# Attention with the bucket mask inside the score product, normalised probabilities and two-tile steps, in front of two feed-forward stages

## The reference

```python
B, H, S, D = q.shape                       # 2, 8, 768, 64
q_bits = (np.einsum('bhsd,dk->bhsk', q, proj) > 0)
k_bits = (np.einsum('bhsd,dk->bhsk', k, proj) > 0)
q_bucket = np.sum(q_bits * powers, axis=-1)
k_bucket = np.sum(k_bits * powers, axis=-1)
mask = q_bucket[:, :, :, None] == k_bucket[:, :, None, :]
scores = np.where(mask, q @ k.T / sqrt(D), -1e9)
scores = scores - np.max(scores, axis=-1, keepdims=True)
attn = np.exp(scores)
attn = attn / (np.sum(attn, axis=-1, keepdims=True) + 1e-09)
x = (attn @ v), heads side by side         # 1536 x 512
h = np.maximum(np.maximum(x @ w1, x @ w2), x @ w3)      # 1536 x 768
y = h @ w_out                                           # 1536 x 512
g = y @ w_in;  g = g * sigmoid(1.702 * g)               # 1536 x 2048
out = g @ w_out2
```

## Time and profile before

| | |
|---|---|
| median of 3 runs | 754.82 us (754.74 to 755.68) |
| span of the profiled execution | 752.0 us, 2.8 below the median of the runs |
| TensorE matmul (PE) busy | 740.9 us, 99% |
| TensorE weight load (PEld) busy | 638.3 us, 85% |
| VectorE (DVE) busy | 362.1 us, 48% |
| ScalarE (ACT) busy | 281.3 us, 37% |
| GpSimd (POOL) busy | 245.6 us, 33% |
| DMA, mean rate | 69 GB/s |
| mean granted clock of TensorE | 0.995 |
| attention stage | from 0 to some 280 us |

### The profile page before, as it was taken

How to read it: one execution, slowest core, us unless ns; L and a number is a source line. 1 busy time by engine, 2 the same in 40 slices (tenths; PEclk the granted TensorE clock), 3 DMA queues, 4 the chain that set the end, 5 groups by cost and what they waited for, 6 DMA issues and landing times.

```text
span 752.0 us, 12394 instructions
## 1 busy us (share of the span) xinstructions
PE 740.9 (99%) x4348; PEld 638.3 (85%) x4348; DVE 362.1 (48%) x794; ACT 281.3 (37%) x586; POOL 245.6 (33%) x230
## 2 busy tenths in 40 slices
PE   6999999999999999999999999999999999999998
PEld 5766777777677669999999999999899899989997
DVE  4988888888888872223222233232222333232222
ACT  3667676666667651111111111322222222222222
POOL 2211111211111152351455242644445445444541
PEclk8999999999999999999999999999999999999999
DMA  4422222243221141201231211212222214222112
GB/s 116 105 64 65 63 64 63 73 96 81 63 63 42 44 138 41 85 22 42 79 111 42 63 41 48 75 59 71 64 56 69 70 43 154 71 70 56 56 42 84
DMA packets 80218, 51.75 MB, mean 69 GB/s; under 512 B 28480, under 2 KB 71488, under 8 KB 80192
## 3 DMA queue, kind: packets, MB, share of 16 engines
q1 hardware_dynamic: 80192, 51.40, 25.1%
HBM read 38.80 MB, written 3.15 MB: 56 GB/s over the span
## 4 chain that ended last, share of the span: by engine, by line
PE 97%; DVE 1%; ACT 1%; DMA 1%; SPq 0%; issue 0%; DVEq 0%
PE psO L811 10%; PE psT L799 10%; PE psS L789 9%; PE psS L881 7%; PE psS L882 7%; PE psS L883 7%; PE psN L883 3%; PE psN L881 3%; PE psN L882 3%; PE psB L882 3%; PE psB L881 3%; PE psB L883 3%; PE psB L754 3%; PE psS L959 2%; PE psS L958 2%; PE psS L957 2%
## 5 line engine op out<-in xcount | busy, mean ns | idle before, releaser
L335 POOL TENSOR_SCALAR w_hi<-w_raw 128x512 fp32r<-128x512 f32 (+2 forms) x84 | 64.3, 766 | 276.1 <-PE psX L959 129.3
L358 POOL TENSOR_TENSOR w_lo<-w_raw,w_hi 128x512 fp32r<-128x512 f32 (+2 forms) x84 | 140.8, 1677 | 7.0
L417 ACT ACTIVATE probs<-masked,neg_max 128x768 f32<-128x768 f32 x96 | 89.8, 936 | 64.2 <-DVE neg_max L566 63.6
L335 POOL TENSOR_SCALAR h_hi<-h_lo 64x768 fp32r<-64x768 f32 x48 | 40.1, 835 | 209.4 <-ACT h_lo L405 204.4
L799 PEld LDWEIGHTS psT<-ident,probs 128*128 128x128 f32 x576 | 62.1, 140 | 47.6 <-issue 44.3
L566 DVE CUSTOM_DVE_ANT_0 masked<-psS,mask 128x768 f32<-128x768 f32 x96 | 91.7, 955 | 18.1 <-PE psS L789 17.7
L881 PE MATMUL psS<-x_hi,w_hi 128*128 128x384 f32 x288 | 96.6, 335 | 0.0
L883 PE MATMUL psS<-x_hi,w_lo 128*128 128x384 f32 x288 | 96.2, 334 | 0.0
L882 PE MATMUL psS<-x_lo,w_hi 128*128 128x384 f32 x288 | 96.2, 334 | 0.0
L789 PE MATMUL psS<-h_hi 128*128 128x384 f32 x384 | 93.0, 364 | 1.6 <-DVE neg_max L566 1.5
L799 PE MATMUL psT<-ident,probs 128*128 128x128 f32 x576 | 83.1, 280 | 1.5 <-ACT probs_t L425 1.5
(11 more groups left out here) (137 smaller groups left out, 1362.2 us busy)
## 6 DMA issues: line engine op xcount, KB each, us to landing
h_hi<-h_lo SPq DMA_DIRECT2D x48, 192.0 KB, 3.9
w_raw<-in_moe_w SPq DMA_DIRECT2D x36, 256.0 KB, 3.5
w_raw<-in_moe_w_in SPq DMA_DIRECT2D x32, 256.0 KB, 2.8
w_raw<-in_moe_w_out SPq DMA_DIRECT2D x32, 256.0 KB, 2.7
v_raw<-in_v SPq DMA_DIRECT2D x16, 192.0 KB, 2.4
w_raw<-in_moe_w_out SPq DMA_DIRECT2D x24, 128.0 KB, 2.4
out<-probs_t SPq DMA_DIRECT2D x12, 256.0 KB, 2.2
w_raw<-in_q SPq DMA_DIRECT2D x15, 192.0 KB, 3.3
```

The lines of the kernel that those rows point to most:

```text
L335: return pool.tensor_scalar(dst, src, 1.0, 1.0, ALU.mult, ALU.mult)
L358: pool.tensor_tensor(w_lo[par][:, c0:c1], w_raw[par][:, c0:c1], f32(w_hi[par][:, c0:c1]), ALU.subtract).then_inc(done, 1)
L417: act.activation(probs[t % 2][:, :], masked[t % 2][:, :, :].rearrange("p a b -> p (a b)"), ACT.Exp, bias=neg_max[t % 2][:, 0:1], scale=-1. ...
```

## The change

The attention stage is written anew; the loops of the feed-forward stages stay as they are.

- **Mask in the product.** The scores' second pass gets, beside the low parts, a one-hot vector of 64 buckets for queries and for keys, the latter scaled by 2^100. `project` is now one bank per head pair: four matmuls (q and k of two heads, two halves of the tokens) as four column tiles of 32. `make_bits` turns it into plus and minus one half, `spread_hot` multiplies by a table of the 64 codes, `make_hot` compares with a threshold. The separate mask, the masked scores in SBUF and the bucket numbers go.
- **Scores and exponential.** `row_max` takes the minimum straight from PSUM, and the exponential reads PSUM. There are two score pairs, `psS[0]` and `psS[1]`; each is free only when its exponential is done.
- **Normalised first.** Per two tiles VectorE makes the inverse sums (`invert_sums`), POOL scales the probabilities in place (`norm`), and only then TensorE turns them. `turn_out`, `normalise` and `turn_x` go: P*V now writes x itself, already turned, for two heads at once (the two heads are the column tiles, three query tiles of each at a time, a "unit").
- **A ring of three PSUM banks** (`psR`) takes everything that is turned or projected, in one order for the whole stage, `ring_order`.
- **Steps of two tiles**, 48 in all, six to a head pair.
- **Stacks.** Each head has four stacked operands (q and k, each with low parts and with one-hot), filled by eight DMAs of 64x768; q and k are split by POOL. SP's queue per head pair: loads of q and k of the next pair, twelve copies of high and low parts, four of one-hot, loads of v.
- POOL splits the first block of feed-forward weights in six pieces in the last pair (`early_split`).

```diff
+    ring_order = [("codes",)]
...
+    for k_ in range(STEPS + 1):
+        p_, st = k_ // 6, k_ % 6
+        if st in (3, 4) and p_ + 1 < PAIRS:
+            ring_order += [("one_hot", 2 * p_ + 2 + st - 3, j) for j in range(2)]
+        if st == 2 and p_ + 1 < PAIRS:
+            ring_order += [("bits", p_ + 1)]
+        if k_ > 0:
+            ring_order += [("probs", i, j) for i in (2 * k_ - 2, 2 * k_ - 1) for j in range(2)]
+        if st < 2 and p_ + 1 < PAIRS:
+            ring_order += [("turn", 2 * p_ + 2 + st, j) for j in range(2)]
...
@@ block.sync @@
-            def stack_qk(m, par):
-                sync.wait_ge(qk_hi_made, 2 * m + 2)
-                sync.dma_start(f32(k_st[par][0:D, :]), f32(qk_hi[D:P, :])).then_inc(qk_stacked[par], 16)
-                sync.wait_ge(qk_lo_made, 2 * m + 2)
-                sync.dma_start(f32(q_st[par][D:P, :]), f32(qk_lo[0:D, :])).then_inc(qk_stacked[par], 16)
-                sync.dma_start(f32(k_swap[par][0:D, :]), f32(qk_lo[D:P, :])).then_inc(k_swapped[par], 16)
+            def load_v(p):
+                if p >= 2:
+                    sync.wait_ge(unit_out, 2 * p - 2)
+                for a in range(2):
+                    sync.dma_start(v_raw[p % 2][a][:, :, :], v_r[2 * p + a, :, :, :]).then_inc(v_loaded[p % 2], 16)
+            def place_hi(m):
+                a = m % 2
+                if m >= 4:
+                    sync.wait_ge(scores_ready, 2 * NT * (m // 2 - 1))
+                sync.wait_ge(qk_hi_made, m + 1)
+                for rows, to, of in ((slice(0, D), Q_LO, slice(0, D)), (slice(D, P), Q_HOT, slice(0, D)),
+                                     (slice(D, P), K_LO, slice(D, P)), (slice(D, P), K_HOT, slice(D, P))):
+                    sync.dma_start(f32(stack(m, to)[rows, :]), f32(qk_hi[a][of, :])).then_inc(hi_placed[a], 16)
...
+            for p in range(PAIRS):
+                if p + 1 < PAIRS:
+                    for m in (2 * p + 2, 2 * p + 3):
+                        load_qk(m)
+                for m in (2 * p, 2 * p + 1):
+                    place_hi(m)
+                    place_lo(m)
+                for m in (2 * p, 2 * p + 1):
+                    place_hot(m)
+                if p + 1 < PAIRS:
+                    load_v(p + 1)
...
@@ block.gpsimd @@
+            for step in range(STEPS):
+                p, st = step // 6, step % 6
+                if st in (1, 2) and p + 1 < PAIRS:
+                    make_qk_hi(2 * p + 1 + st)
+                    make_qk_lo(2 * p + 1 + st)
+                norm(2 * step)
+                norm(2 * step + 1)
+                if p == PAIRS - 1:
+                    early_split(st)
...
@@ block.scalar @@
+            for step in range(STEPS + 1):
+                p, st = step // 6, step % 6
+                if step < STEPS:
+                    exp_tile(2 * step)
+                    exp_tile(2 * step + 1)
+                if step >= 6 and step % 3 == 0:
+                    x_hi_unit(step // 3 - 2)
+                if step > 0:
+                    copy_turned(2 * step - 2)
+                    copy_turned(2 * step - 1)
+                if st < 2 and p + 1 < PAIRS:
+                    for j in range(2):
+                        copy_qk(2 * p + 2 + st, j)
...
@@ block.vector @@
+            for step in range(STEPS + 1):
+                p, st = step // 6, step % 6
+                if step < STEPS:
+                    row_max(2 * step)
+                    row_max(2 * step + 1)
+                    if st in (3, 4) and p + 1 < PAIRS:
+                        for j in range(2):
+                            make_hot(2 * p + st - 1, j)
+                    invert_sums(step)
+                    if st == 2 and p + 1 < PAIRS:
+                        make_bits(p + 1)
+                if step >= 6 and step % 3 == 0:
+                    x_lo_unit(step // 3 - 2)
+                if step > 0:
+                    copy_turned(2 * step - 2)
+                    copy_turned(2 * step - 1)
...
@@ block.tensor @@
+            for step in range(STEPS + 1):
+                p, st = step // 6, step % 6
+                if step < STEPS:
+                    scores(2 * step)
+                    scores(2 * step + 1)
+                if st in (3, 4) and p + 1 < PAIRS:
+                    spread_hot(2 * p + st - 1)
+                if step >= 4:
+                    u, part = (step - 4) // 3, (step - 4) % 3
+                    for c in (2 * part, 2 * part + 1):
+                        times_values(u, c)
+                if st == 2 and p + 1 < PAIRS:
+                    project(p + 1)
+                if step > 0:
+                    turn_probs(2 * step - 2)
+                    turn_probs(2 * step - 1)
+                if st < 2 and p + 1 < PAIRS:
+                    turn_qk(2 * p + 2 + st)
```

## The result

| | before | after |
|---|---|---|
| median of the runs | 755.07 us (754.74 to 755.68, 4 runs) | 812.43 us (810.98 to 815.31, 4 runs) |
| ratio, 95% interval | | 1.077 (1.074 to 1.079) |
| span of the profiled execution | 752.0 us | 811.7 us (its own time 813.54 us) |
| mean granted clock of TensorE | 0.995 | 0.947 |
| first row minimum starts | 13.38 us | 27.94 us |

The change costs 57 us, 7.7%. The forecast was 799 us, in a range of 757 to 820: the sign and the mechanism were right, and the measured time lies 13.4 us above the forecast. The page of the kernel after, parts 1, 2 and 4: busy us and share of each engine, the span in 40 slices of 20.3 us, and the chain that ended last by engine.

What follows compares the result with a forecast made beforehand. Attention was to be bound by the three-bank ring loop and late copies through SyncE, no longer by TensorE: 23.95 + 251.0 + 32.8 + 9 + 6.7 + 472.8 = 796.3 us of span, plus 2.8, 799 us; range 757 to 820.

Steps and rivals of the forecast that it cites:

- steps to the last minimum, no stall: Attention steps from first minimum to the last step's first minimum, without stalls or clock term: 251.0 us.
- last minimum to feed-forward: End of attention: sums, two scalings and the last split piece before the first feed-forward product, 6.7 us.
- span to median: Offset added because the profiled execution's span of 752.0 lies 2.8 us under the median of 754.82.
- signs named: TensorE share 70 to 75%, 4 to 6 us idle at pairs, SP's v wait, 4.9 us steps, feed-forward at 315 to 325.
- The ring's loop: Attention steps: fourth turned bank waits for ScalarE's copy behind two exponentials; 4.86 us plain step, 32.8 a pair.
- The stall: Pair starts: copies queue on SyncE behind the v load; 6.0 us at pairs 2 to 6, 2.8 before 7, 32.8 total.
- The clock: TensorE at low clock after each stall: 1.5 us for each of six, 9 in all (0 to 18).
- The start: Before first scores, 15 more DMAs: 21.2 by issue, 24.2 by transfer, 22.8 taken; first minimum at 23.95 us.
- Projection: Attention's four projection matmuls as four column tiles at once, 0.8 us; 1.5 if two by two.
- Rival 1: Copies land in time at pair starts and only the ring loop counts: 757 us; chance 0.07.
- Rival 2: TensorE keeps the pace in attention, saving 5.1 us a pair: 724 us; chance 0.05.
- Rival 3: POOL's subtraction holds VectorE's small sums operation in attention, 26 us more: 825 us; chance 0.06.

Runs made afterwards that it cites:

- experiment 1: Kernel after, with each pair's load of v moved behind its own copies in SP's queue (first pair's v stays first): 751.47 us, 0.996 of the kernel before.
- experiment 6: On top of experiment 5, the next step's first scores issued between the turns of tiles A and B, minimum and exponential moved along: 736.81 us, 0.975.
- experiment 4: Kernel after, with 36 filler matmuls before the wait for the one-hot copies at pairs 2 to 7, keeping TensorE busy: 809.83 us (one run).
- experiment 2: On top of experiment 1, at the start head 0's copies first, then head 1's, then next q and k loads, then v: 748.40 us, 0.992.
- experiment 5: Experiment 2 with q and k loads of the third head right behind the first head's copies, the fourth's behind the second's: 745.79 us, 0.987.
- experiment 8: Experiment 6 without the addition of 1e-9 to the row sums, the reciprocal reading the sums directly: 732.54 us, 0.970 of the kernel before.
- experiment 7: Kernel after with the interleaved steps alone, v load and start left as they were: 814.87 us (one run).
- experiment 3: Kernel after, but from the third pair on each stack copy moves half its columns, same number and order of DMAs: 778.79 us (one run).

## Why the prediction was right, and where its size was off

From first minimum to first minimum of the last step the kernel after takes 331.94 - 27.94 = 304.0 us; 251.0 + 32.8 + 9 = 292.8 was predicted. With the start, the tail and the offset the 13.4 us are accounted for (a stall is what the step in front of it takes above 4.6):

| term of the sum | predicted | measured | difference |
|---|---|---|---|
| first row minimum | 23.95 | 27.94 | +4.0 |
| steps to the last minimum, no stall | 251.0 | 241.8 (experiment 1, 27.41 to 269.21) | -9.2 |
| six stalls | 32.8 | 54.5 | +21.7 |
| clock, step behind a stall | 9 | 6.4 | -2.6 |
| first pair, against experiment 1 | in the steps | 1.3 | +1.3 |
| last minimum to feed-forward | 6.7 | 6.65 | 0 |
| feed-forward | 472.8 | 473.1 | +0.3 |
| span to median | 2.8 | 0.7 | -2.1 |

- **What bounds it.** Right, and shown: with the wait for P*V out of the way of the copies (experiment 1) 61 us go, and when the ring's loop is opened (experiment 6) 9 more. Neither TensorE nor any engine's busy time bounds the attention stage of the kernel after. Of the signs named, the released bank, SP's wait for P*V and the idle time ended by stack copies were there (4 to 6 us named; measured before the third to the seventh pair are 6.2 to 6.8 in front of the second pass of the scores, and some 2 in front of the first). Two came out beside their range: TensorE is busy for 78% of the stage (262.69 of 338.60 us; 70 to 75 named), and the feed-forward stage starts at 338.59 (315 to 325).
- **The ring's loop.** Right in every link, a little high in each. A pair was put at 32.8 and is 31.3: steps of 6.03, 5.47, 5.45, 4.97, 4.79 and 4.60 against 6.33, 5.74, 5.74, 5.25, 4.86 and 4.86. Step 3 shows it: of 0.28 us, 0.11 is the scores to the minimum (0.98 instead of 1.09), 0.10 the two exponentials (0.89 and 0.87 instead of 0.93), the rest the copies. The intervals of rows 3 were taken where TensorE set the pace and nothing waited for them; that this made them longer is a guess.
- **The stall: the term that failed in size.** "I take 0.8 each", for 20 DMAs, was the step. The row it was taken from already said 0.875: two copies in seven columns of 0.25 us, and the discount for partly filled columns was not borne out. Measured are 0.88 each, and nearly 22 have to pass, because with SP ahead of the transfers the second head's one-hot copies move together with the first's. That makes 19.1 us instead of 16. Release (20.8 against 20.3) and handoff add 0.7, and 0.75 of landing falls away. A round is 41.85 us (100.76 to 142.61) where 38.8 plus the clock's 1.5 was predicted, so only 1.6 too low. But the stall is what remains above the pair, and the pair itself is 1.5 shorter: 9.2 to 10.0 us for each of five, not 6.0, and 6.1 before the last, not 2.8. Of the 21.7 us some 9 are that shift from the steps and no new cost: in a round bound by transfers, faster steps turn into longer waiting.
- **The clock.** Right in kind: the step behind each stall is 0.6 to 1.8 us longer, mean 1.1 where 1.5 was put, and in experiment 4 that went, in all six rounds, when TensorE was kept busy.
- **The start.** Same error as in the stall. The last one-hot copy of the first head was issued at 19.40 and landed 7.45 later, where 3 to 4 was the pattern: the queue behind it was full. Mixed by issue and by transfer, my 22.8 lay between the two, and transfer (24.2) was nearer. Experiments 2 and 5 show that it was mendable: the first minimum comes at 19.
- **Projection** in 0.85 us as four column tiles (taken: 0.8), and the feed-forward stage of 473.1 us (taken: 472.8): both right.
- **Rival 1**, copies in time, 757: not what the change does, but what experiment 1 makes of it (751.5: the shorter steps, less the later start).
- **Rival 2**, TensorE keeps pace, 28.4 a pair and 724: it needed the loop opened as well as the copies in time. Experiment 8 is that kernel, with 29.0 to 30.1 a pair and 732.5.
- **Rival 3**, POOL holds VectorE. Not in the kernel after: of its 48 sums one was held, the only one that came while POOL subtracted.

The group of the sums in the kernel after (min/median/max ns), and the long one in its timeline:

```profile
L596 DVE TENSOR_SCALAR guarded<-sums x48: 158/169/1812, 31.2 to 334.8; 128x2 f32<-128x2 f32 x48
```

The long one:

```profile
34.39 1.80 POOL L374 TENSOR_TENSOR w_lo<-w_raw,w_hi 128x768 fp32r<-128x768 f32 x1
34.40 1.81 DVE L596 TENSOR_SCALAR guarded<-sums 128x2 f32<-128x2 f32 x1 [1.08 <-ACT probs L476]
```

The mechanism was real, and only the moments at which POOL subtracted kept the kernel from it. With the two tiles interleaved (experiments 6 and 7) it came up in each pair but the last, and taking the addition away from experiment 6 was worth 4.3 us.

The 732.5 us come from four edits on the kernel after: the load of v moved (61.0), the start (5.7 in two), the two tiles interleaved (9.0), the small addition dropped (4.3). What of the 29.0 us a pair is left to win was not tried, nor was the interleaving without the addition under the stall.

## What to carry to other kernels

On a queue that issues in order, ask of each waiting transfer what stands behind it and when that is due: a load that could have waited held up everything the next head pair needed, and moving one call was worth 61 us, while the rewriting with all its mendings gained 22. When a queue is issued faster than it is transferred, price a group of transfers by all the bytes in flight and not by those in front of the one that is awaited. And fix the longest loop first: here the same interleaving was worth nothing under the stall and 9 us without it.

## What was not expected of the hardware

- **Transfers in flight share the engines.** A stack copy (64x768, 192 KB, SBUF to SBUF) lands 3.0 to 4.5 us after its issue in the kernel before, but with a median of 5.2 to 5.5 in the kernel after, and 7.45 at its start, where more are in flight at once. With half of the bytes (experiment 3) the one-hot copies landed 2.2 us after their issue. The 22 transfers of a round moved at some 220 GB/s (98% of 4.33 MB in 19.1 us).
- **A tiny operation can be held for the whole of a POOL operation, and its neighbour not.** The addition on 128x2 went from 0.17 to 1.68 and 1.81 us beside POOL's subtraction, in one case begun 0.01 us behind it. The reciprocal of the same shape was not: six of them in experiment 6 and seven in experiment 8 began while that subtraction ran, and none of the 48 in either took over 168 ns. The Trainium skill, "GPSIMD Engine Reference", section "Key points", names contention for VectorE operations in a mode that uses both ports, and "VectorE: DVE Perf Modes", section "What auto-detection actually checks", gives that mode to operations with a single source and a destination in SBUF whose outer dimensions are even or equal. The addition is one, and the trace agrees with its being held. Why the reciprocal is spared no run here shows.
- **The clock comes back late.** After a wait of 6.5 us the granted clock stayed at 0.50 (1.2 GHz) for about 4 us of continuous work (142 to 146), and that step took 1.1 us longer than one without a wait ahead.
